# A fused attention and feed-forward kernel: where the vector engine's convolution taps, two small matches and one exponent per half pair stand in each engine's program

## The reference

```python
q_bits = (np.einsum('bhsd,dk->bhsk', q, proj) > 0)      # 6 bits per token, keys alike
mask = q_bucket[:, :, :, None] == k_bucket[:, :, None, :]
scores = np.where(mask, scale * q @ k.T, -1e9)
attn = exp(scores - max); attn = attn / (sum + 1e-09)
x = attn @ v                                             # then heads side by side: (2, 768, 512)
gate_pre += conv_w[k] * xp[:, k:k + S, :]                # k = 0..4
x = (1 / (1 + exp(-gate_pre))) * (x @ w_val) @ w_out
# second block: mix with the previous token, relu, square, w_v, gate by w_r
```

## Time and profile before

| what | value |
|---|---|
| median of 3 runs | 512.54 us (512.49 to 512.74) |
| the profiled execution | 510.61 us, of which the span of the profile is 508.8 us |
| PE busy | 481.3 us, 95% |
| DVE busy | 354.3 us, 70% |
| ACT busy | 283.4 us, 56% |
| POOL busy | 271.1 us, 53% |
| chain that ended last | PE 70%, DVE 15%, issue 7%, ACT 6%, POOL 2% |
| granted TensorE clock | 0.999 of full speed |

### The profile page before, as it was taken

The page is one execution under the profiler, slowest core; times in us unless marked ns, Lnnn a source line. Parts: engine busy times, 40 slices in busy tenths (PEclk is TensorE's granted clock), DMA queues, the critical chain, the costliest instruction groups (busy, mean ns, idle before and its releaser), DMA issues.

```text
span 508.8 us, 9512 instructions
## 1 busy us (share of the span) xinstructions
PE 481.3 (95%) x3564; PEld 408.0 (80%) x3564; DVE 354.3 (70%) x604; ACT 283.4 (56%) x601; POOL 271.1 (53%) x259
## 2 busy tenths in 40 slices
PE   8679989999899998999999999999999999999997
PEld 7556666666566665666777999999999999999997
DVE  3676697796978969788858798597398298325211
ACT  3696776868768687786664543354245145144140
POOL 5693663936549274494136674548247347445240
PEclk9999999999999999999999999999999999999999
DMA  5121030311202112020022000100000100100101
GB/s 197 32 82 49 11 119 17 100 47 41 89 17 100 47 60 72 16 68 17 17 84 84 1 2 1 43 1 12 31 2 2 43 1 1 43 0 2 43 2 43
DMA packets 10575, 20.83 MB, mean 41 GB/s; under 512 B 1696, under 2 KB 6816, under 8 KB 10528
## 3 DMA queue, kind: packets, MB, share of 16 engines
q1 hardware_dynamic: 10224, 19.94, 11.9%
q10 hardware_dynamic: 304, 0.27, 0.2%
HBM read 17.06 MB, written 3.15 MB: 40 GB/s over the span
## 4 chain that ended last, share of the span: by engine, by line
PE 70%; DVE 15%; issue 7%; ACT 6%; POOL 2%; DMA 1%; DVEq 0%; ACTq 0%; POOLq 0%
PE ps L679 27%; PE ps L687 11%; PE ps L667 11%; PE ps L629 10%; PE ps L643 8%; ACT q L440 3%; DVE negmax L803 3%; DVE gate L846 3%; DVE pt L810 2%; DVE k L795 1%; DVE tmp_a L916 1%; DMA raw_q<-qT 1%; PE ps L604 1%; ACT probs L448 1%; DVE tmp_b L914 1%
## 5 line engine op out<-in xcount | busy, mean ns | idle before, releaser
L803 DVE TENSOR_REDUCE negmax<-ps 128x1 f32<-128x768 f32 x96 | 91.8, 956 | 48.6 <-PE ps L629 47.8
L629 PE MATMUL ps<-k,q 128*128 128x384 f32 x384 | 92.2, 362 | 12.5 <-ACT probs L448 12.0
L448 ACT ACTIVATE probs<-ps,negmax 128x768 f32<-128x768 f32 x96 | 86.6, 902 | 17.2 <-DVE negmax L803 15.4
L643 PE MATMUL ps<-ident,probs 128*128 128x128 f32 x576 | 82.2, 275 | 4.4 <-DVE pt L810 4.1
L629 PEld LDWEIGHTS ps<-k,q 128*128 128x128 f32 x384 | 63.0, 189 | 28.0 <-ACT probs L448 22.8
L643 PEld LDWEIGHTS ps<-ident,probs 128*128 128x128 f32 x576 | 67.0, 140 | 14.2 <-DVE pt L810 5.5
L667 PE MATMUL ps<-pt,vals 128*64 128x384 f32 x384 | 68.8, 494 | 0.8 <-DVE x L836 0.8
L456 ACT ACTIVATE pt<-ps 128x384 f32<-128x384 f32 x96 | 46.7, 487 | 31.0 <-PE ps L643 28.8
L406 POOL TENSOR_TENSOR h_lo<-tmp_b,h_hi 128x256 fp32r<-128x256 f32 x48 | 38.5, 807 | 46.0 <-ACT h_hi L546 46.0
L846 DVE SCALAR_TENSOR_TENSOR gate<-x,conv_sb,gate 128x256 f32<-128x256 f32 x96 | 60.9, 634 | 2.4
L810 DVE COPY pt<-ps 128x384 f32<-128x384 f32 x96 | 52.2, 544 | 3.5 <-PE ps L643 3.5
(11 more groups left out here) (88 smaller groups left out, 1161.5 us busy)
## 6 DMA issues: line engine op xcount, KB each, us to landing
w_raw<-w SPq DMA_DIRECT2D x8, 640.0 KB, 4.0
raw_q<-qT SPq DMA_DIRECT2D x8, 384.0 KB, 3.0
raw_k<-kT SPq DMA_DIRECT2D x8, 384.0 KB, 4.4
vals<-v SPq DMA_DIRECT2D x16, 192.0 KB, 2.3
out<-w_raw SPq DMA_DIRECT2D x24, 128.0 KB, 1.7
w_raw<-w SPq DMA_DIRECT2D x4, 512.0 KB, 3.2
codes_f<-codes ACTq DMA_DIRECT2D x1, 256.0 KB, 5.7
proj_bd<-proj ACTq DMA_DIRECT2D x2, 1.5 KB, 3.9
```

What stands on the lines that cost most here:

```text
L448: act.activation(probs[par][:, :], score[par], ACT.Exp, bias=negmax[:, t:t + 1], accum_out=sums[:, t, 0:1]).then_inc(exp_done, 1)
L629: last = pe.matmul(ps[:, 2 * par + half, 0:HALF], qq[h][:, q], kk[h][:, half * HALF:(half + 1) * HALF], start=first, stop=not first)
L643: last = pe.transpose(tbank[u][:, k * P:(k + 1) * P], probs[g % 2][:, kt * P:(kt + 1) * P], ident[:, :])
L803: dve.tensor_reduce(negmax[:, t:t + 1], score[g % 2], AX.XY, ALU.max, negate=True).then_inc(max_done, 1)
```

## The change

Three tables of steps are changed.

- Exponent: in steps 3 and 6 (of all pairs but the last) ACT takes the exponent of tile g + 2 before it makes the one-hot queries, and no longer behind them at the start of the next step. Burst steps did this already.
- Matches: match 1 moves from the end of step 4 into step 5, between the transposes and the product. Match 3 moves from the end of step 7 into step 8, to the same place. Matches 0 and 2 stay behind the products of steps 2 and 5.
- Taps: of six taps per pair, two stood in step 8 and four in step 11. Now three stand in step 11, and three in step 2 of the next pair, so step 2 of the last pair has three as well. The last pair's own taps in steps 5 and 8 stay.

```diff
-MATCH_STEPS = {2: 0, 4: 1, 5: 2, 7: 3}
+MATCH_AHEAD, MATCH_BEHIND = {5: 1, 8: 3}, {2: 0, 5: 2}
 HOTQ_STEPS = {3: 0, 6: 1}
...
+    if i > 1 and t == 2:
+        return range(6 * (i - 1) - 3, 6 * (i - 1))
     if i == PAIRS - 1:
         return {5: range(36, 38), 8: range(38, 40)}.get(t, ())
-    if i and t == 8:
-        return range(6 * (i - 1), 6 * (i - 1) + 2)
     if i and t == 11:
-        return range(6 * (i - 1) + 2, 6 * i)
+        return range(6 * (i - 1), 6 * (i - 1) + 3)
     return ()
...
-def product_step(g):
-
-    return g >= KT and g % KT in PV_STEPS
+def ahead_step(g):
+    return 0 <= g < PAIRS * TILES - 2 and \
+        (g >= KT and g % KT in PV_STEPS or g < LAST * TILES and g % TILES in HOTQ_STEPS)
...
-                if g + 1 < PAIRS * TILES and not product_step(g - 1):
+                if g + 1 < PAIRS * TILES and not ahead_step(g - 1):
                     exp_tile(g + 1)
                 first_half_up(g)
-                if g + 2 < PAIRS * TILES and product_step(g):
+                if ahead_step(g):
                     exp_tile(g + 2)
...
                 transposes(g)
+                if i < LAST and t in MATCH_AHEAD:
+                    match(i + 1, MATCH_AHEAD[t])
                 if tt in PV_STEPS and head:
                     product(head - 1, PV_STEPS[tt])
...
-                    if t in MATCH_STEPS:
-                        match(i + 1, MATCH_STEPS[t])
+                    if t in MATCH_BEHIND:
+                        match(i + 1, MATCH_BEHIND[t])
```

More of the change, by code:

```diff
@@ L18 @@
 PAIRS = BATCH * HEADS // 2
+LAST = PAIRS - 1
 NHEADS = 2 * PAIRS
@@ L227, in build @@
         LO, HI = slice(0, DH), slice(DH, P)
-        LAST = PAIRS - 1
         def x_tokens(c, first=HALO):
```

## The result

The first measurement gave 506.58 us for the change (median of 4, 505.96 to 507.48) and 512.51 us for the kernel before (median of 4, 510.19 to 512.74), a ratio of 0.9896 with a 95% interval of 0.9862 to 0.9929. Two more jobs timed the same change at 0.9917 (0.9904 to 0.9929) and 0.9941 (0.9925 to 0.9957). Over all jobs the kernel before has a median of 510.8 us (64 executions, 509.75 to 512.74), and the change one of 507.2 us (14 executions, 505.96 to 508.46). So the change makes the kernel faster by about 3.6 us, 0.7%. The profiled execution went from 510.61 to 507.48 us.

What follows compares the result with a forecast made beforehand. PE was taken as the bound, with gaps in steps 5 and 8 (exponent) and 10 and 11 (DVE). Terms -5.5 + 1.84 + 1.1 = -2.6 us took 512.54 to 509.9 us, range 507.6 to 512.0.

Steps and rivals of the forecast that it cites:

- Part 1: Step 8 of six pairs: taps leave, scores of steps 10 and 11 come 1.56 us apart; -5.5 us.
- Part 2: Step 2, pairs 2 to 6: three taps fit into DVE's idle time while POOL is idle; cost nothing.
- Part 3: Step 2 of the last pair: POOL's `w_lo` and `x_low` hold the taps, the next maximum is late; +1.84 us, once.
- Part 4: Steps 3 to 8: wait for the first-half copy replaces that for the exponent; +0.18 us per pair, +1.1 for six.
- the last pair is spared: Rival: no loss from step 2 taps in the last pair, 508.1 us; gain of 4 us and more, together 0.13.
- the gain go back in the burst steps: Rival: part 4 costs 0.6 us per pair, 3.7 in all, sum 0.0, 512.5 us; chance 0.15 for within 0.2%.
- the kernel become slower: Rival: ACT's chain bounds steps 5 and 8, 513.6 us, or POOL holds step 2 taps in other pairs; together 0.10.
- A gain as large as 4 us and more: Rival outcome: last pair spared (508.1 us), or part 4 at its low bound (507.5 us); chance together 0.13.

Runs made afterwards that it cites:

- queries later: The change, but exponents of steps 4 and 7 in their old order and one-hot queries behind the first-half copy (steps 4 and 7): 497.56 us, ratio 0.9749.
- exponents as before: The change, but the exponents of steps 4 and 7 stand behind the one-hot queries as in the kernel before: 508.37 us, ratio 0.9956 to the kernel before.

## Why the prediction was right or wrong

**The number was wrong.** It said 509.9 us, 507.6 to 512.0; measured were 506.58, and 507.2 over all jobs. The step that failed is the last of the sum: "The median of the runs is 1.93 above the profiled one, so the median becomes 512.54 - 2.6 = 509.9 us." That sum takes 1.93 us, the distance between three unprofiled executions and one profiled, for a property of the kernel. It is none: of 64 executions five lie above 512.3, and those three are among them. The median over all is 510.8, nearly the time of the profiled execution (510.61). What put those three there stays open. For its like the prediction said 508.0, and the profiled execution took 507.48. From 510.8 the same sum would have given 508.2, which is still 1.0 above 507.2; that rest is the terms, which were 0.9 too small. So of the 3.3 us between 509.9 and the first 506.58, some 1.7 are the base, 1.0 the terms, and 0.6 the four executions of the change, which lay that far below its median over all jobs. The range was made of the terms of the sum alone, and held nothing for the base.

**The terms, in the loop (240.33 to 236.83, 3.5 us less, for 2.6).**
- Part 1, taps out of step 8: -5.5 predicted. The six distances of step 10 sum to 15.05 us before and 9.39 after: -5.66. Right. (With exponents and matches moved alone the sum is 14.61, so 0.4 of this depends on where the taps meet POOL.)
- Part 2, taps in step 2: nothing predicted, and DVE is idle for 0.54 us behind them. Right.
- Part 3, last pair: +1.84 predicted, +1.61 measured. The mechanism is right, and shown by moving `x_low` alone. By the Trainium skill (SBUF — State Buffer, "Who interferes with whom") the later one of the two is blocked, and with this the run agrees: the same taps took 3.47 us beside `x_low` and 1.46 without. POOL did let a tap in between its two instructions, as the earlier trace rows had it, which cost `x_low` 0.18 us (2.56 for 2.38). The size was off by 0.23: I counted 3.91 us from the idle of DVE to its next maximum (240.67 to 244.58), and it was 3.66 (235.95 to 239.61). The difference is the third tap: the maximum began 0.19 us behind the end of the second one (239.42), where I had counted 0.42.
- Part 4, exponents and matches: +1.1 predicted, +0.07 to +0.09 us per pair measured, 0.5 in six pairs, which is the largest of the misses in the terms. The mechanism is right, and "queries later" confirms it: with the queries out of the row, the wait for the copy was gone. In pair 6 the product of step 5 comes 5.68 us behind the scores of step 3, where it was 5.54, 0.14 late for 0.18, and that of step 8 is early by 0.05 (5.69 for 5.74, from the scores of step 6) where I had nothing. Mis-sized was the queries' start behind the exponent: I took 0.95 between two rows, and it was 0.89 (209.01 to 209.90), the lower one. The match costs 0.17 there (0.91 from transposes to product in "exponents as before", for 0.74 without a match), more than the 0.10 that I took, but I had counted the transposes at their whole 0.82, where 0.74 from start to start was due, so that the two together came out nearly right (0.92 for 0.94).

**The rivals.** That the last pair is spared did not come true. Nor did the gain go back in the burst steps, nor did the kernel become slower. A gain as large as 4 us and more had 0.13, and the first measurement looked like it, by the base.

## What to carry to other kernels

Look on each engine for the row of instructions between a result and the engine that waits for it, and move what nobody waits for out of this row, not around inside it: an exponent ahead of the queries, with the matches in the burst steps, cost 0.5 us, and the queries behind the copy gave nearly 10. Instructions of DVE with two inputs in SBUF belong where POOL is idle, also in the last turn of a loop, which here had other work under it. And before a time is worked out from a few executions, ask how far executions of this kernel lie apart: here by 3.0 us (509.75 to 512.74), with a change of 3.6.

## What the runs showed of the hardware

TensorE's granted clock fell for some 3.4 us in pair 0 in three of fifteen profiled executions, 0.1 to 1.3 us behind a wait of PE of 1.54 or 1.91 us, and four score matmuls took up to 1.68 us instead of 1.00; pair 0 became 0.6 to 1.0 us longer. Whether it falls differs between executions of the same program: the same waits stand in profiles without a fall, and by the mean granted clock 28 of 60 executions of the kernel before had one. With eight more transposes at either of two waits of pair 0, none of sixteen had.

Two taps with two inputs in SBUF took 3.47 us where POOL's `w_lo` and `x_low` stood under them in a row, and 1.46 us with `x_low` elsewhere. The start of the loop varied from 14.63 to 16.70 us, with the landing of the first loads.
